# Attention in front of two feed-forward networks: row maxima by single banks, uneven pieces of the product with v over two banks, another way to add the two halves of the output, and a start with two query tiles

## What is computed

```
q_pool = q.reshape(B, H, S // 2, 2, D).mean(axis=3)
scores = scale * np.matmul(q_pool, k.transpose(0, 1, 3, 2))
scores = scores - np.max(scores, axis=-1, keepdims=True)
attn = np.exp(scores)
attn = attn / (np.sum(attn, axis=-1, keepdims=True) + 1e-09)
x = np.matmul(attn, v)            # then (tokens, heads * dims)
g = P(x @ w_in) / Q(x @ w_in)     # a cubic over a quadratic with abs
x = g @ w_out
xn = x / rms(x) * rms_g
out = (silu(xn @ w_gate) * (xn @ w_val)) @ w_out2
```

## Time and profile before

| | |
|---|---|
| median of 3 runs | 710.39 us (709.19 to 710.42) |
| the profiled execution | 711.4 us, span of its instructions 709.6 us |
| TensorE busy | 692.3 us, 98% of the span |
| VectorE, ScalarE, GpSimd busy | 536.1, 413.8, 392.0 us |
| matrix products of the networks in the chain that ended last | L598 32.2%, L639 22.6% |
| of the attention in that chain | L491 (scores) 12.5%, L515 (products with v) 10.6%, L500 (transposes) 9.5% |
| mean granted TensorE clock | 1.000 |

### The profile page before, as it was taken

One profiled execution on the slowest core, in us unless ns is written; L12 is line 12 of the kernel. 1 busy time (PEld: TensorE's weight loads), 2 busy tenths in 40 slices (PEclk: granted clock), 3 DMA queues, 4 the chain that ended last, 5 costly groups with the idle time before them and its releaser, 6 DMA issues.

```text
span 709.6 us, 12014 instructions
## 1 busy us (share of the span) xinstructions
PE 692.3 (98%) x4067; PEld 638.4 (90%) x4067; DVE 536.1 (76%) x999; ACT 413.8 (58%) x877; POOL 392.0 (55%) x363
## 2 busy tenths in 40 slices
PE   6899999999999998899999999999999999999998
PEld 4899999999999998799999999988999999999996
DVE  5899999999999997988988988987554344444442
ACT  4687777777777778988877888873521111111110
POOL 5756585855658664978978888866543512000000
PEclk9999999999999999999999999999999999999999
DMA  8342222224220011011101101111220200000012
GB/s 289 105 151 85 85 90 85 93 83 142 86 88 17 1 60 60 1 61 60 50 11 60 60 1 60 59 61 60 91 87 1 84 36 0 1 1 1 0 45 89
DMA packets 18027, 44.35 MB, mean 62 GB/s; under 512 B 1984, under 2 KB 2880, under 8 KB 17856
## 3 DMA queue, kind: packets, MB, share of 16 engines
q1 hardware_dynamic: 17696, 43.39, 18.3%
q10 hardware_dynamic: 288, 0.39, 0.2%
HBM read 41.42 MB, written 2.36 MB: 62 GB/s over the span
## 4 chain that ended last, share of the span: by engine, by line
PE 89%; ACT 4%; DVE 2%; POOL 1%; DMA 1%; issue 1%; SPq 0%; POOLq 0%; ACTq 0%
PE hb L598 32%; PE ob L639 23%; PE sc L491 13%; PE pv_ps L515 11%; PE sc L500 10%; DMA vrawA<-in_v 1%; ACT den L765 1%; ACT num L767 1%; ACT lin L768 1%; PE pv_ps L533 0%; PE misc L533 0%; ACT hb L784 0%; POOL kqB L389 0%; DVE xb L1014 0%; ACT h L766 0%
## 5 line engine op out<-in xcount | busy, mean ns | idle before, releaser
L598 PE MATMUL hb<-xt_hi,wi_hi 128*128 128x384 f32 x336 | 113.9, 339 | 4.0 <-DVE gt_lo L981 3.8
L715 ACT ACTIVATE pt_hi<-sc 128x384 fp32r<-128x384 f32 x192 | 80.4, 492 | 56.5 <-PE sc L500 56.5
L598 PE MATMUL hb<-xt_lo,wi_hi 128*128 128x384 f32 x336 | 113.1, 337 | 0.0
L598 PE MATMUL hb<-xt_hi,wi_lo 128*128 128x384 f32 x336 | 112.8, 336 | 0.0
L639 PE MATMUL ob<-wo_hi,gt_hi 128*128 128x512 f32 x252 | 98.5, 391 | 1.5 <-DVE gt_lo L981 1.5
L639 PE MATMUL ob<-wo_lo,gt_hi 128*128 128x512 f32 x252 | 99.2, 394 | 0.0
L639 PE MATMUL ob<-wo_hi,gt_lo 128*128 128x512 f32 x252 | 99.0, 393 | 0.0
L887 DVE TENSOR_TENSOR pt_lo<-sc,pt_hi 128x384 fp32r<-128x384 f32 x192 | 94.5, 547 | 0.0
L701 ACT ACTIVATE prob<-sc,neg_max 128x1152 f32<-128x1152 f32 x72 | 89.5, 1243 | 2.6 <-DVE neg_max L875 2.6
L500 PE MATMUL sc<-ident,prob 128*128 128x128 f32 x648 | 82.6, 273 | 0.2 <-ACT prob L701 0.2
L500 PEld LDWEIGHTS sc<-ident,prob 128*128 128x128 f32 x648 | 74.9, 140 | 3.1 <-ACT prob L701 0.4
(11 more groups left out here) (130 smaller groups left out, 1683.4 us busy)
## 6 DMA issues: line engine op xcount, KB each, us to landing
wraw<-in_moe_w_out SPq DMA_DIRECT2D x7, 1024.0 KB, 5.2
qrawB<-in_q SPq DMA_DIRECT2D x8, 576.0 KB, 3.9
krawB<-in_k SPq DMA_DIRECT2D x8, 576.0 KB, 4.8
wraw<-in_moe_w_in SPq DMA_DIRECT2D x4, 1024.0 KB, 5.0
qrawA<-in_q SPq DMA_DIRECT2D x7, 576.0 KB, 3.9
krawA<-in_k SPq DMA_DIRECT2D x7, 576.0 KB, 4.9
wraw<-in_moe_w_gate SPq DMA_DIRECT2D x3, 1024.0 KB, 5.2
wraw<-in_moe_w_val SPq DMA_DIRECT2D x3, 1024.0 KB, 5.2
```

Source lines behind the costliest of these rows:

```text
L598: ins = nc.tensor.matmul(bank[:, 0:BLOCK], w[i][:, d, col], x[j][:, d, BLOCK * nb:BLOCK * nb + BLOCK], start=d == 0 and n == 0, stop=d == ...
L715: ins = nc.scalar.activation(pt[buf][0][:, 3 * c:3 * c + 3, c0:c0 + P], src, ACT.Copy)
```

## The change

- **Row maximum.** Each of the three banks has a reduction of its own, behind its own `qk_done` count; a small reduction makes the minimum of three negated maxima. The factor 1/16 is now put into the queries when they are split (GpSimd writes a scaled copy for it, one instruction more for each image and pair), so exp and maximum carry no scale.
- **Products with v.** Two tables, `PV_AT` and `PV_LATE`, say which of a group's 18 products stand in which step ahead of the scores, and which behind them. Groups alternate between the banks `pv_ps` and `misc`. The transposed parts `pt` lie in one ring of 640 columns, so tile 4 needs three copies and not six.
- **Combination.** ScalarE copies the first two parts of a combined pair to `o_rows` (two copies of 512 columns); GpSimd adds the halves ahead of `divide`. VectorE keeps the third part.
- **Start.** The first transfer brings 256 queries, VectorE splits them, `qk(1)` stands behind `qk(0)` and ahead of 7 products that nobody reads. SyncE waits for the middle third of the keys before it issues q, k and v of image B.

The core of the diff:

```diff
-EARLY = P
-WARM = (4, 6)
+EARLY = 2 * P
+WARM = (4, 7)
-TILE_AT = {0: (1, 64), 1: (1, 192), 2: (0, 0), 3: (0, 128), 5: (1, 64), 6: (1, 192), 7: (0, 0), 8: (0, 128)}
+PT_COL = (384, 512, 0, 128, 256, 384, 512, 0, 128)
+PV_AT = {0: ((3, 0, 9),), 1: ((3, 9, 18),), 3: ((0, 0, 10),), 4: ((0, 10, 18),), 5: ((1, 2, 11),), 6: ((1, 11, 18),), 7: ((2, 2, 10),), 8: ((2, 10, 18),)}
+PV_LATE = {4: (1, 0, 2), 6: (2, 0, 2)}
...
+        def pv_bank(g, last):
+            return pv_ps if last else (pv_ps, misc)[g % 2]
...
             sp.dma_start(qraw[0][:, :, EARLY:ROWS], q[0, 0, :, :, EARLY:ROWS]).then_inc(first_q[1], 16)
+            sp.wait_ge(first_k[1], 16)
             load_kq(1, 0)
...
-                    nc.gpsimd.tensor_scalar(q_part(x, 0), qraw[x][:, 0], 1.0, 0.0, ALU.mult, ALU.add).then_inc(s, 1)
+                    nc.gpsimd.tensor_scalar(q_part(x, 0), qraw[x][:, 0], SCALE, 0.0, ALU.mult, ALU.add).then_inc(s, 1)
+                    nc.gpsimd.tensor_scalar(qraw[x][:, 1], qraw[x][:, 0], SCALE, 0.0, ALU.mult, ALU.add).then_inc(s, 1)
...
-                flat = o_rows[:].rearrange("p a t d -> p (a t) d")[:, 0:TILES]
+                rows = o_rows[:, 0:TILES - 1]
+                nc.gpsimd.tensor_tensor(rows[:, :, 0:HEAD_DIM], rows[:, :, 0:HEAD_DIM], rows[:, :, HEAD_DIM:], ALU.add).then_inc(rows_sum, 1)
...
-                    if c != 1:
-                        ins.then_inc(qk_done, 1)
+                    ins.then_inc(qk_done, 1)
...
                     turn(i, h, s)
-                    if i in (0, 1) and not is_first(h):
-                        pv(3, h - 1, i)
+                    for g, j0, j1 in PV_AT.get(i, ()):
+                        if g < 3:
+                            pv(g, h, j0, j1)
+                        elif not is_first(h):
+                            pv(g, h - 1, j0, j1)
...
-                    if i in (3, 4):
-                        pv(0, h, i - 3)
-                    if i in (5, 6):
-                        pv(1, h, i - 5)
-                    if i in (7, 8):
-                        pv(2, h, i - 7)
...
                         qk(i + 2 - TILES, h + 1, s)
+                    if i in PV_LATE:
+                        g, j0, j1 = PV_LATE[i]
+                        pv(g, h, j0, j1)
...
             qk(0, 0, 0)
+            qk(1, 0, 1)
             for _ in range(WARM[1]):
                 nc.tensor.matmul(pv_ps[:, 0:KBANK], kq[0][:, 0], k_part(0, 0, KBANK), start=True, stop=True)
-            qk(1, 0, 1)
...
-                                     bias=neg_max[:, s:s + 1], scale=SCALE, accum_out=sums[:, (s + i) % 2, i:i + 1]).then_inc(exp_done, 1)
+                                     bias=neg_max[:, s:s + 1], accum_out=sums[:, (s + i) % 2, i:i + 1]).then_inc(exp_done, 1)
...
+            def rows_copy(h, part, par):
+                if part == 0:
+                    act.wait_ge(rows_done, h + 1)
+                act.wait_ge(comb_t, h * 3 + (part + 1))
+                nc.scalar.activation(o_rows[:, 4 * part:4 * part + 4].rearrange("p t d -> p (t d)"), part_bank(part, par, False)[:], ACT.Copy).then_inc(comb_evac, 1)
...
+                    if i == 2 and not is_first(h):
+                        rows_copy(h - 1, 0, 1 - par)
+                        rows_copy(h - 1, 1, 1 - par)
...
-                dve.wait_ge(qk_done, (h * 9 + i) * 2 + 1)
-                nc.vector.tensor_reduce(neg_part[:, s, 0:1], sc[s][:, 0, 0:KBANK], AX.X, ALU.max, negate=True).then_inc(part_done, 1)
-                if between:
-                    between()
-                dve.wait_ge(qk_done, (h * 9 + i) * 2 + 2)
-                nc.vector.tensor_reduce(neg_part[:, s, 1:2], sc[s][:, 1:3, 0:KBANK], AX.XY, ALU.max, negate=True).then_inc(part_done, 1)
-                dve.wait_ge(part_done, (h * 9 + i) * 2 + 2)
-                nc.vector.tensor_scalar(neg_max[:, s:s + 1], neg_part[:, s, 0:1], neg_part[:, s, 1:2], SCALE, ALU.min, ALU.mult).then_inc(max_done, 1)
+                n = (h * 9 + i) * 3
+                for c in range(3):
+                    dve.wait_ge(qk_done, n + (c + 1))
+                    nc.vector.tensor_reduce(neg_part[:, s, c:c + 1], sc[s][:, c, 0:KBANK], AX.X, ALU.max, negate=True).then_inc(part_done, 1)
+                    if c == 0 and between:
+                        between()
+                dve.wait_ge(part_done, n + 3)
+                nc.vector.tensor_reduce(neg_max[:, s:s + 1], neg_part[:, s], AX.X, ALU.min).then_inc(max_done, 1)
...
-                    if i == 2 and not is_first(h):
-                        gather(h - 1, 1 - par, 0)
-                        gather(h - 1, 1 - par, 1)
```

More of the change, by code:

```diff
@@ L124, in build @@
         o_sb = sbuf(att, "o_sb", [P, TOKENS])
-        o_rows = sbuf(att, "o_rows", [P, 3, 4, HEAD_DIM])
-        pt = [[sbuf(att, f"pt{s}_{x}", [P, KEY_TILES, GROUP], F32R) for x in ("hi", "lo")] for s in range(2)]
+        o_rows = sbuf(att, "o_rows", [P, TILES, 2 * HEAD_DIM])
+        pt = [sbuf(att, f"pt_{x}", [P, KEY_TILES, 2 * GROUP], F32R) for x in ("hi", "lo")]
         v2 = [sbuf(att, f"v2{x}", [P, KEY_TILES, 2, HEAD_DIM], F32R) for x in "AB"]
@@ L213, in build @@
         comb_evac = sem("comb_evac")
+        comb_tail = sem("comb_tail")
+        rows_sum = sem("rows_sum")
         rows_done = sem("rows_done")
@@ L440, in _ @@
             pool.wait_ge(s, 1)
-            nc.gpsimd.tensor_scalar(q_part(0, 0, EARLY, ROWS), qraw[0][:, 0, rest], 1.0, 0.0, ALU.mult, ALU.add).then_inc(s, 1)
-            pool.wait_ge(s, 2)
-            nc.gpsimd.tensor_tensor(q_part(0, 1, EARLY, ROWS), qraw[0][:, 0, rest], q_part(0, 0, EARLY, ROWS).bitcast(F32), ALU.subtract).then_inc(s, 3)
+            nc.gpsimd.tensor_scalar(q_part(0, 0, EARLY, ROWS), qraw[0][:, 0, rest], SCALE, 0.0, ALU.mult, ALU.add).then_inc(s, 1)
+            nc.gpsimd.tensor_scalar(qraw[0][:, 1, rest], qraw[0][:, 0, rest], SCALE, 0.0, ALU.mult, ALU.add).then_inc(s, 1)
+            pool.wait_ge(s, 3)
+            nc.gpsimd.tensor_tensor(q_part(0, 1, EARLY, ROWS), qraw[0][:, 1, rest], q_part(0, 0, EARLY, ROWS).bitcast(F32), ALU.subtract).then_inc(s, 3)
             split(1, 0, 0, 0)
@@ L478, in qk @@
                 tile = [i if x == 0 else (MIXED if i == MIXED else i - MIXED - 1) for x in (0, 1)]
-                early = is_first(h) and i == 0
+                early = is_first(h) and i < 2
                 if not early:
                     for x in heads:
-                        pe.wait_ge(kq_split[x], h * 5 + 5)
+                        pe.wait_ge(kq_split[x], h * 6 + 6)
                 for c in range(3):
@@ L501, in turn, with pv @@
                     ins.then_inc(pt_t, 1)
-            def pv(g, h, half):
+            def pv(g, h, j0, j1):
                 x, last_tile, buf, c0, n, _ = GROUPS[g]
-                if half == 0:
+                bank = pv_bank(g, is_last(h) and g == 3)
+                if j0 == 0:
                     pe.wait_ge(pt_lo, (h * 9 + (last_tile + 1)) * 3)
                     pe.wait_ge(v_split[x], h * 2 + 2)
-                    if not (is_first(h) and g == 0):
-                        pe.wait_ge(o_evac, h * 4 + g)
-                        if g == 0:
-                            pe.wait_ge(comb_evac, h * 3 - 2)
-                for j in range(KEY_TILES * half, KEY_TILES * half + KEY_TILES):
+                    if is_last(h) and g == 3:
+                        pe.wait_ge(o_evac, h * 4 + 3)
+                    elif not (is_first(h) and g < 2):
+                        pe.wait_ge(o_evac, h * 4 + (g - 1))
+                        if g < 2:
+                            pe.wait_ge(comb_evac, h * 2 + (g - 1))
+                for j in range(j0, j1):
                     kt, e = j // 2, j % 2
-                    ins = nc.tensor.matmul(pv_ps[:, 0:n], v2[x][:, kt].rearrange("p a d -> p (a d)"), pt[buf][e][:, kt, c0:c0 + n],
+                    ins = nc.tensor.matmul(bank[:, 0:n], v2[x][:, kt].rearrange("p a d -> p (a d)"),
+                                           pt[e][:, kt, GROUP * buf + c0:GROUP * buf + c0 + n],
                                            start=j == 0, stop=j == 2 * KEY_TILES - 1)
-                if half:
+                if j1 == 2 * KEY_TILES:
                     ins.then_inc(pv_done, 1)
@@ L722, in o_copy @@
                     act.wait_ge(comb_t, h * 3)
-                nc.scalar.activation(o_sb[:, o0:o0 + n], pv_ps[:, 0:n], ACT.Copy).then_inc(o_evac, 1)
+                nc.scalar.activation(o_sb[:, o0:o0 + n], pv_bank(g, is_last(h) and g == 3)[:, 0:n], ACT.Copy).then_inc(o_evac, 1)
             def pair(h, par):
@@ L900, in gather @@
                 n = len(PARTS[part])
-                if part == 0:
+                if not is_last(h) or part == 0:
                     dve.wait_ge(rows_done, h + 1)
@@ L904, in gather @@
                 both = part_bank(part, par, is_last(h))[:, 0:P * n].rearrange("p (t a d) -> p t d a", a=2, d=HEAD_DIM)
-                nc.vector.tensor_reduce(o_rows[:, part, 0:n], both, AX.X, ALU.add).then_inc(comb_evac, 1)
```

(1 more changed line is left out.)

60 lines of the change are left out of this document (26 added, 34 removed).

## The result

| | before | with the change |
|---|---|---|
| median | 710.40 us (709.19 to 711.24, 6 runs) | 706.45 us (705.54 to 707.42, 6 runs) |
| ratio, 95% interval | | 0.9946 [0.9933, 0.9959] |
| profiled execution, its span | 711.4, 709.6 us | 705.85, 704.1 us |
| transposes of tile 3, pair 0, start at | 24.51 | 25.80 |
| of tile 3, pair 7 | 242.85 | 238.27 |

What follows compares the result with a forecast made beforehand. VectorE's round was taken to bound four of nine steps, TensorE the rest. Loop -7.0 and start +1.2 gave -5.8 from 711.4, 705.6; less 1.0 to the median, 704.6 us, range 702.8 to 708.0 for 8 in 10.

Steps and rivals of the forecast that it cites:

- What bounds: Attention loop: VectorE's round of 3.31 us limits four steps of nine, TensorE the rest; score products wait 1.06 us a pair.
- the row maximum: VectorE's reductions, one per bank: its round falls from 3.31 to 3.05 us, leaving TensorE the longest loop at 3.10.
- Uneven pieces: TensorE's products with v: no gain of their own; two more starts a pair at 0.07 us each add 1.1 us.
- The sum for the loop: Attention pairs: 8.1 us of waits removed, 1.1 added for the pieces, net -7.0 us; bounds -8.1 to 0.
- Combination: Step 2, adding a pair's halves: moving work off VectorE gains nothing; ScalarE's copies and GpSimd's extra work cost nothing.
- Start: First tiles, pair 0: image B's key chain on GpSimd gets longer and starts later, costing 1.2 us (-0.8 to +1.6).
- the first rival: TensorE's wait of 4.6 us for image B's keys at the start halves its clock, costing 1.9: 706.5 us; chance 0.27.
- From the profiled execution to the median: Whole kernel: profiled execution 705.6 us, less the 1.0 by which the earlier one exceeded its median, gives 704.6.
- the stated range: Whole kernel's median: 702.8 to 708.0 us for 8 in 10, with the clock and most of the half-waits added.
- Reductions by bank: Slower rival, VectorE's row maximum: reductions do not overlap, 0.59 apart, round 3.41 us, total 720.0 us; chance 0.06.
- Half of the waits: Rival in the attention loop: three near-equal engine loops meet, 3.5 us of the gain go, 708.1 us; chance 0.15.
- The early keys: Rival at the start: middle keys land at about 5 us, start gains 0.8, total 702.6 us; chance 0.06.

## Why the prediction was right and wrong

- **What bounds, and the row maximum: right.** Waits of 1.06 a pair inside the score groups, removed by a shorter round of VectorE. Predicted pair 30.3, measured 30.25; predicted round 3.05, measured 2.99. Undoing the maximum alone costs 5.6 us and brings the waits back.
- **Uneven pieces: right in sign and nearly in size.** 0.14 a pair predicted as a cost, 0.10 measured (30.25 against 30.15), and the wait left in step 4 is as large. The sum for the loop was -7.0; the pairs and the last pair's tiles give -6.34 - 0.34 = -6.7.
- **Combination: mis-sized.** "VectorE has time: nothing" priced VectorE by step 2, where that holds. The two reductions of 0.68 make the following step late, which has no slack with the shorter round: 0.14 in step 3, 0.1 of the pair.
- **Start: this step failed, twice.** It put the middle keys at "6.95 as now, the nearest row". They came at 5.5 with the change, at 5.25 without its hold and at 5.97 in the kernel before: the row was that of one execution. GpSimd's chain was to start at 13.0 and started at 11.90, and the start without the clock cost 0.16 and not 1.2. What made up for it was the clock, the first rival: a wait of 4.6 predicted, 4.08 measured, 1.9 predicted, 1.6 measured in the profiled execution and 2.0 to 2.4 in the medians by the run with TensorE kept busy. The mechanism was right; that the size was near is in part luck, for the 1.9 was taken from the launch, whose granted clock is recorded as 1.00 (last section). Forecast and rival differed only in whether the clock falls, and I gave the fall 0.27 against 0.46, because no wait of that trace had done it; the second profile of the kernel before shows one that did. The Trainium skill, TensorE: Matmul & The Clock Gate, Part 1, has the rule (idleness throttles); this trace agrees, with 0.50 granted behind a stand of 4.08; behind the stand of 3.25 in the last section the clock did not fall.
- **From the profiled execution to the median: this failed too.** The sum gave 705.6 and the profiled execution took 705.85, by luck: the start was 1.0 too dear and the networks, which were to change nothing, 0.6 shorter; the loop gained 0.3 less and the clock cost 1.6 that the sum did not have. The 1.0 that I then took off, because the execution of before lay that far above its median, did not carry over: that of after lies 0.6 below its own. Executions of the change at a mean clock of 0.998 took 705.5 to 706.0, those at 0.994 and 0.995 took 706.6 to 707.4; what one kernel's profiled execution has over its median did not carry over to the other's. The median is inside the stated range because the clock was put into it.
- **Other rivals.** Reductions by bank do overlap, 0.47 apart. Half of the waits did not stay (0.1 a pair in step 4). The early keys came, but did not bring 702.6: an earlier first tile only lengthens the wait for image B.

## What to carry to other kernels

Split a reduction along the boundaries at which its input becomes ready, and price it by the distance between starts (0.47 here), not by the drawn length of one (0.55); that alone decided this change. Before an early chain is made earlier, look at what its engine waits for next: here that lengthened TensorE's stand to 4.08 us, with the low clock behind it in both profiles, while reordering the late chain on another engine (keys ahead of v) gained 5.6 us of the median, 4.8 between the profiled executions. A gain that came with several edits is worth taking apart: two of the edits here were losses, the uneven pieces and the start.
